# Linear attention and two gated MLP layers on one core: zeros, the order of step 0 and 1, alternating PSUM banks, and a first sum moved to GpSimd

## The reference

```python
kv = einsum('bhsd,bhse->bhde', k, v)              # 4 x 8 heads, 576 tokens, 64 wide
out = einsum('bhsd,bhde->bhse', q, kv)
rms = sqrt(mean(out * out, axis=-1) + 1e-06)
x = (out / rms * g_norm)  ->  [2304 tokens, 512]
h = x @ w_in1;  x = (h * sigmoid(1.702 * h)) @ w_out1     # w_in 512 x 2048, w_out 2048 x 512
h = x @ w_in2;  out = softplus(h) @ w_out2
```

## Time and profile before

| | |
|---|---|
| median of 3 runs | 817.93 us (817.62 to 819.13) |
| profiled execution | 818.39 us, span of instructions 816.6 us |
| TensorE matmul busy | 805.2 us, 99% of the span |
| TensorE weight load busy | 734.2 us |
| VectorE busy | 588.9 us |
| ScalarE busy | 425.0 us |
| GpSimd busy | 223.0 us |
| chain that ended last | TensorE 92%, VectorE 3%, ScalarE 2% |

### The profile page before, as it was taken

The page is one execution under the profiler, slowest core; times in us unless marked ns, Lnnn a source line. Parts: engine busy times, 40 slices in busy tenths (PEclk is TensorE's granted clock), DMA queues, the critical chain, the costliest instruction groups (busy, mean ns, idle before and its releaser), DMA issues.

```text
span 816.6 us, 12377 instructions
## 1 busy us (share of the span) xinstructions
PE 805.2 (99%) x4604; PEld 734.2 (90%) x4604; DVE 588.9 (72%) x1029; ACT 425.0 (52%) x809; POOL 223.0 (27%) x263
## 2 busy tenths in 40 slices
PE   8989999999999999999999999999999999999998
PEld 7978999999999999999998888898888988989886
DVE  3779767687665786665678777888767889766774
ACT  3773332334221233223246776788767678766765
POOL 4888987304421403254501401100000000000000
PEclk9999999999999999999999999999999999999999
DMA  9936547426455462756642525224433322452402
GB/s 358 405 158 236 213 143 280 159 116 217 159 219 203 154 238 91 246 200 250 231 171 101 206 102 205 107 90 150 164 126 119 152 91 101 159 180 90 149 33 77
DMA packets 24426, 139.78 MB, mean 171 GB/s; under 512 B 2224, under 2 KB 6960, under 8 KB 17200
## 3 DMA queue, kind: packets, MB, share of 16 engines
q1 hardware_dynamic: 24224, 138.95, 46.6%
q10 hardware_dynamic: 144, 0.07, 0.0%
HBM read 104.92 MB, written 34.08 MB: 170 GB/s over the span
## 4 chain that ended last, share of the span: by engine, by line
PE 92%; DVE 3%; ACT 2%; issue 1%; DMA 1%; SPq 0%; ACTq 0%; DVEq 0%
PE ps L640 42%; PE ps L705 23%; PE ps L713 16%; PE ps L710 8%; PE ps L583 1%; DMA kv_in_sb<-k_v 1%; PE ps L566 1%; DVE xs_f L984 1%; DVE gs_f L1013 1%; PE ps L602 0%; DVE ex L1066 0%; DVE rms L953 0%; PE ps L588 0%; DVE gs_f L1069 0%; ACT fix L819 0%
## 5 line engine op out<-in xcount | busy, mean ns | idle before, releaser
L640 PE MATMUL ps<-xs,w_in 128*128 128x384 f32 x2016 | 409.5, 338 | 2.3 <-DVE gs_f L1013 2.0
L640 PEld LDWEIGHTS ps<-xs,w_in 128*128 128x128 f32 x2016 | 356.4, 188 | 27.7 <-issue 4.0
L705 PE MATMUL ps<-w_out,gs 128*128 128x512 f32 x864 | 226.0, 393 | 0.0
L1013 DVE TENSOR_TENSOR gs_f<-ps,gs_f 128x384 f32<-128x384 f32 x240 | 133.2, 555 | 113.7 <-PE ps L640 112.2
L705 PEld LDWEIGHTS ps<-w_out,gs 128*128 128x128 f32 x864 | 160.0, 188 | 23.9 <-issue 0.5
L713 PE MATMUL ps<-gs,w_out 128*128 128x512 f32 x576 | 148.2, 392 | 0.0
L713 PEld LDWEIGHTS ps<-gs,w_out 128*128 128x128 f32 x576 | 105.6, 188 | 16.4
L809 ACT ACTIVATE lg<-gs_f 128x384 f32<-128x384 f32 x73 | 38.3, 526 | 123.2 <-DVE gs_f L1013 122.1
L487 POOL TENSOR_TENSOR w_in<-w_in_f,w_in 128x256 fp32r<-128x256 f32 x112 | 94.1, 876 | 29.1 <-ACT w_in L849 28.9
L844 ACT CAST gs<-gs_f 128x384 fp32r<-128x384 f32 x96 | 48.9, 509 | 67.7 <-DVE gs_f L1073 66.4
L710 PE MATMUL ps<-gs,w_out 128*128 128x256 f32 x576 | 83.9, 281 | 0.1
(11 more groups left out here) (64 smaller groups left out, 576.8 us busy)
## 6 DMA issues: line engine op xcount, KB each, us to landing
w_in<-w_kept SPq DMA_DIRECT2D x40, 1792.0 KB, 7.3
w_kept<-w_in SPq DMA_DIRECT2D x16, 1792.0 KB, 10.8
w_in_f<-w_in SPq DMA_DIRECT2D x16, 512.0 KB, 4.1
w_out_f<-w_out SPq DMA_DIRECT2D x16, 512.0 KB, 9.0
kv_in_sb<-k_v SPq DMA_DIRECT2D x8, 640.0 KB, 10.2
kv_in_sb<-k_v SPq DMA_DIRECT2D x8, 576.0 KB, 11.9
q_sb<-q_t SPq DMA_DIRECT2D x16, 288.0 KB, 10.2
out<-xy SPq DMA_DIRECT2D x18, 256.0 KB, 7.8
```

Of the source, the lines that this page charges most:

```text
L640: mm = nc.tensor.matmul(ps[:, bank, 0:HALF], w[:, wp, W_OF[k], cols], xs[:, k, xp, t], start=(new and t == 0 and (wp, xp) == (HI, HI)), st ...
L705: mm = nc.tensor.matmul(ps[:, acc_bank(1, j), 0:DM], g[:, j * P:(j + 1) * P], w, start=new, stop=done)
L1013: nc.vector.tensor_tensor(to, bank, other, ALU.add).then_inc(added, 1)
```

## The change

1. After raw_output(0) TensorE multiplies five more zeros.
2. Banks alternate: in odd steps BANK_A and BANK_B change places (bank_a, bank_b). P1 of step m then waits only for C21_ADD of step m - 1, and P6 for C12_ADD.
3. product(1, P1) is issued between turn(15) and product(0, P3). The counts of prod_done follow (products_done, step_done).
4. hidden(0, C21) moves on ScalarE ahead of the last gain, and on VectorE the whole gate of C21 stands ahead of C12_ADD in step 0.
5. x's first sums: T1 on VectorE behind unit 8 (it needs x_made 6), T3 on GpSimd (first_t3), T2 on VectorE behind unit 10, where it waits for T3, and T4 behind unit 11.
6. GpSimd's queue: x_early(B21) ahead of w_sums(1), then w_high(1), w_low(1), x_early(B22), first_t3, x_early of T1, T3, T2, T4. The wait for the split of step 0's C21 stands ahead of w_sums(2) instead of behind it.

```diff
         def products_done(m, k):
-            place = {P2: P6, P6: P2}.get(k, k) if m == 0 else k
+            place = {P2: P6, P6: P2, P3: PRODUCTS}.get(k, k) if m == 0 else -1 if (m, k) == (1, P1) else k
             return PRODUCTS * m + place + 1
-        X_EARLY = (B11, B21, B22, T3, T2, T4, T1)
+        X_EARLY = (B11, B21, B22, T1, T3, T2, T4)
+        X_EARLY_SUMS = (T1, T2, T4)
+            def first_t3():
+                a, b, op = x_sum_of(0, T3)
+                nc.gpsimd.tensor_tensor(x_sum(0, T3), a, b, op).then_inc(t3_early, 1)
             x_early(B11)
+            x_early(B21)
             w_sums(1)
-            x_early(B21)
             w_high(1)
             w_low(1)
-            for slot in X_EARLY[2:]:
+            x_early(B22)
+            first_t3()
+            for slot in X_EARLY[3:]:
                 x_early(slot)
             w_out_low(0, 0)
+            pool.wait_ge(g_split, C21 + 1)
             w_sums(2)
-            pool.wait_ge(g_split, C21 + 1)
             w_high(2)
-                bank = BANK_B if k in (P6, P7, P4) else BANK_A
+                bank = bank_b(m) if k in (P6, P7, P4) else bank_a(m)
                     if m > 0:
-                        pe.wait_ge(added, ADDS * (m - 1) + C12_ADD + 1)
+                        pe.wait_ge(added, ADDS * (m - 1) + C21_ADD + 1)
+                if k == P6 and m > 0:
+                    pe.wait_ge(added, ADDS * (m - 1) + C12_ADD + 1)
                 raw_output(u)
+                if u == 0:
+                    zeros(5)
             turn(UNITS - 1)
+            product(1, P1)
             product(0, P3)
@@ ScalarE
+                if u == UNITS + 1:
+                    hidden(0, C21)
                 if u >= TURN_LAG:
                     gain(u - TURN_LAG)
@@ VectorE
-                if slot == T2:
+                if slot == T2 and ci == 0:
+                    dve.wait_ge(t3_early, 1)
+                elif slot == T2:
                     dve.wait_ge(x_raw_made, x_raws(ci, T3))
-                if u == 2 * PAIRS + 1:
-                    dve.wait_ge(x_made, 2 * PAIRS)
-                    raw_x(0, T3)
+                if u == 2 * PAIRS:
+                    dve.wait_ge(x_made, PAIRS + 2)
+                    raw_x(0, T1)
+                if u == 2 * PAIRS + 2:
                     raw_x(0, T2)
-                if u == 2 * PAIRS + 2:
+                if u == 2 * PAIRS + 3:
                     raw_x(0, T4)
-                if u == 2 * PAIRS + 3:
-                    raw_x(0, T1)
                 if m == 0:
                     gate_split(m, C11)
-                    add(m, C12_ADD)
                 if phase:
                     softplus(m, C21)
                 else:
-                    gate_product(m, C21)
-                    if m > 0:
-                        gate_split(m, C21)
-                if m > 0:
-                    add(m, C12_ADD)
+                    gate(m, C21)
+                add(m, C12_ADD)
                 if ends:
                     low_x(ci + 1, T2)
-                if m == 0:
-                    gate_split(m, C21)
```

More of the change, by code:

```diff
@@ L153, in build @@
         x_raw_made = sem("x_raw_made")
+        t3_early = sem("t3_early")
         x_hi_made = sem("x_hi_made")
@@ L234, in build, with bank_a, bank_b, step_done @@
         P1_UNIT, P2_UNIT = 10, 12
+        def bank_a(m):
+            return BANK_B if m % 2 else BANK_A
+        def bank_b(m):
+            return BANK_A if m % 2 else BANK_B
         def products_done(m, k):
-            place = {P2: P6, P6: P2}.get(k, k) if m == 0 else k
+            place = {P2: P6, P6: P2, P3: PRODUCTS}.get(k, k) if m == 0 else -1 if (m, k) == (1, P1) else k
             return PRODUCTS * m + place + 1
+        def step_done(m):
+            return max(products_done(m, k) for k in range(PRODUCTS))
         def split_buffer(d):
@@ L302, in x_raws @@
         def x_raws(ci, slot):
-            return 4 * ci + X_RAW_ORDER.index(slot) + 1
+            if ci == 0:
+                return X_EARLY_SUMS.index(slot) + 1
+            return len(X_EARLY_SUMS) + 4 * (ci - 1) + X_RAW_ORDER.index(slot) + 1
         def x_his(ci, slot):
@@ L399, in load_raw @@
                     if last is not None:
-                        sp.wait_ge(prod_done, PRODUCTS * (last + 1))
+                        sp.wait_ge(prod_done, step_done(last))
                     sp.wait_ge(w_stored, 16 * ((last if last is not None else d - 1) + 1))
@@ L738, in _ @@
                 for k in range(PRODUCTS):
-                    product(m, k)
+                    if (m, k) != (1, P1):
+                        product(m, k)
                     down(m - 1, came, shares(m)[k])
@@ L787, in first_product @@
                     wait_down(act, m - 2)
-                nc.scalar.copy(hid(m, C21), ps[:, BANK_A, 0:HALF]).then_inc(t1_made, 1)
+                nc.scalar.copy(hid(m, C21), ps[:, bank_a(m), 0:HALF]).then_inc(t1_made, 1)
             def keep_c11():
@@ L801, in hidden @@
                     act.wait_ge(prod_done, products_done(m, P2))
-                    h = ps[:, BANK_A, 0:HALF]
+                    h = ps[:, bank_a(m), 0:HALF]
                 else:
@@ L916, in _ @@
                     round_x(ci + 1, T3)
-                hidden(m, C21)
+                if m > 0:
+                    hidden(m, C21)
                 if ends:
@@ L991, in add @@
             def add(m, which):
-                a, b = ps[:, BANK_A, 0:HALF], ps[:, BANK_B, 0:HALF]
+                a, b = ps[:, bank_a(m), 0:HALF], ps[:, bank_b(m), 0:HALF]
                 p1 = hid(m, C21)
@@ L1039, in hidden_of @@
             def hidden_of(m, tile):
-                return ps[:, BANK_A, 0:HALF] if tile == C11 and m > 0 else hid(m, tile)
+                return ps[:, bank_a(m), 0:HALF] if tile == C11 and m > 0 else hid(m, tile)
             def gate(m, tile):
```

## The result

| | before | after |
|---|---|---|
| median | 817.78 us (817.58 to 819.13, 8 runs) | 822.12 us (819.31 to 823.34, 8 runs) |
| ratio, with its 95% interval | | 1.0044 (1.0032 to 1.0057) |
| profiled execution | 818.39 us, span 816.6 | 822.84 us, span 821.0 |
| VectorE busy, GpSimd busy | 588.9, 223.0 us | 583.6, 225.6 us |

By the medians the change costs 4.3 us, not the 2.3 of the forecast; it lands near the 821.8 of the first rival. The ratio is not the quotient of the medians (1.0053) but an estimate from all executions; it puts the cost at 3.6 us, with 2.6 to 4.7 as its interval. The spans of the two profiled executions differ by 4.4 us, which is where the places can be read.

The account below looks back on a forecast made before the run. Only matmul time bounds TensorE from 64 us on, so edits count in the first 64 us or where another engine stops it. 0.4 us gained up to down(0), 2.7 lost at down(1): +2.3 on 817.93 makes 820.2, range 818.0 to 823.0.

Parts of the forecast that it names:

- rival 1: At down(1): the clock falls in the new TensorE wait of some 2 us; +3.9, 821.8 us, chance 0.22.
- Zeros: First stage: five more zeros hold the clock, 1.6 us saved, but transfers let unit 8 gain at most 0.55.
- Rival 4: First stage: the zeros don't hold the clock, x_made 4 not earlier, 0.6 more; +2.9, 820.8 us, chance 0.08.
- Wait (b): Attention: three raw_output waits for VectorE's scale, 1.8 us together; not saved but replaced, P6 1.1 us later.
- GpSimd in the first stage: Attention: GpSimd idles ahead of B21, then becomes the bound; P6 at 52.05 instead of 50.94, 1.1 us later.
- Products: Up to down(0): products' order gains 1.5 us, less GpSimd's 1.1; down(0) at 62.95 instead of 63.38, 0.4 gained.
- T0: End of step 0's gates: the moment C21 is split, forecast at 62.9 us against 63.3 before.
- GpSimd behind T0: From T0 to down(1): 2.97 us of sums precede a 15.17 us chain; down(1) +1.8 to +2.8, taken as +2.3.
- Rivals 2: At down(1): no wait if GpSimd's collisions stay under 0.4 us; -0.4, 817.5 us, chance 0.07.
- rival 3: Attention: GpSimd isn't the bound, T0 3.3 us earlier, sums behind T0 still cost 2.7; -0.6, 817.3 us, chance 0.07.
- the two together: Attention and down(1): GpSimd isn't the bound and no wait at down(1); -3.5, 814.4 us, chance 0.06.
- if half clock follows the wait: Behind down(1)'s forecast TensorE wait of 2 to 3 us: a sign that would show the forecast wrong.

Follow-up runs that it names:

- e6_zeros_only: The kernel before with the five zeros and nothing else; 818.06 us, ratio 1.0001.
- e2_b21_back: The changed kernel with w_sums(1) ahead of x_early(B21) again in GpSimd's queue; 818.89 us, ratio 1.0003.
- e1_sums_back: The changed kernel with w_sums(2) put back ahead of the wait for C21's split; 818.68 us, ratio 1.0005.
- e8_zeros_products: The changed kernel with GpSimd's queue and x's first sums as before, keeping zeros, alternating banks, P1 ahead of P3 and C21 ahead; 817.08 us, ratio 0.9985.
- e4_fill: The changed kernel with 13 matmuls of unread result in TensorE's wait ahead of down(1); 820.35 us, ratio 1.0025.
- e5_only_sums_late: The kernel before with only the wait for C21's split moved ahead of w_sums(2); 820.78 us, ratio 1.0041.
- e10_fill_both: The changed kernel with filler matmuls in both new waits, 11 ahead of raw_output(13) and 13 ahead of down(1); 819.89 us, ratio 1.0020.
- c_after: The changed kernel run again as it is, beside other experiments on one chip; 822.01 us, ratio 1.0040 against the kernel before.
- e3_both_back: The changed kernel with w_sums(1) ahead of B21 and w_sums(2) ahead of the wait for C21's split again; 816.01 us, ratio 0.9973.

## Why the forecast was right in its places and short in its size

**Zeros: right.** 0.41 us of waiting is left of 1.69, the rows behind it are at full speed (1.16 for the 1.96 of the earlier trace rows), and unit 8 starts at 26.26 where 26.25 was said. The granted clock of the 12th us is 1.00 where it was 0.50:

```profile
12.00:13.00 1.00, 1.00 (x16) 0.88 (x16) 0.84 (x2) 0.23 (x2) 1.00 (x1) 1.00 1.07 421
```

That the transfers leave 0.55 of the 1.6 in the trace is shown by e6_zeros_only; in the median it is 0.2. Rival 4 fell.

**Wait (b) replaced, not saved: right.** VectorE stands still for T3, and its own row for the next sum is

```profile
42.24 1.55 DVE L1020 TENSOR_TENSOR xs_f<-xs_f,xy 128x768 f32<-128x768 f32 x1 [2.21 <-POOL xs_f L529]
```

TensorE waits 1.96 us at raw_output(13) instead of three times for 1.8. e2_b21_back shows the cause: with the old order of GpSimd's queue the wait is gone.

**GpSimd in the first stage: right.** Forecast and trace: B21 at 25.0 (24.79), T3's sum done at 42.5 (40.38 + 1.82 = 42.20), its price 1.8 (1.82), T1's low part at 45.9 (43.06 + 2.40 = 45.46), T2's low part at 52.0 (49.58 + 1.81 = 51.39). P6 at 52.05 came true as 52.07, but not for the stated reason alone: in this execution GpSimd was done 0.7 us before, and TensorE was itself late, with raw_output(13) at the slower clock. In e1_sums_back, at full clock, P6 starts at 51.73 behind GpSimd's subtraction. So the reason holds at full clock, 0.3 us earlier than said, and the fall of the clock filled the difference. The chain was priced well because each item of it had a row of its own kind.

**Products: right.** P5 was said for 58.5 and starts about a product behind 57.24, by estimate at 58.3. T0 was said for 62.9; the split of C21 is

```profile
61.94 0.56 DVE L1093 TENSOR_TENSOR gs<-gs_f,gs 128x384 fp32r<-128x384 f32 x1
```

so T0 is 62.50, and down(0) starts at 62.60 after 0.38 us (62.95 after 0.4 was said). e8_zeros_products confirms a gain from this order, 1.3 us with the zeros, where the forecast counted 0.4 in all because GpSimd's 1.1 was taken off it.

**GpSimd behind T0: right in its chain, with some luck in its time.** The chain ended at 81.21 where 81.1 was said: it began 0.4 earlier and was 0.5 longer, since w_sums(2) took 3.63 (62.58 to 66.21) instead of 2.97, taking turns with VectorE. The wait is 2.53 (2.4), down(1) starts 2.07 later than before, inside the 1.8 to 2.8. (The forecast's own chain, 81.1, gives +1.9; it took 2.3, the middle of its bounds.) That it lies inside is in part luck: about 0.5 of the 2.07 is the fall of the clock in attention, for which the forecast had no term, and in e4_fill, where that fall is missing, down(1) starts 1.57 later. There T0 is at 62.0, 0.9 earlier than said. e1_sums_back and e5_only_sums_late show the cause from both sides, once by undoing the edit and once by doing it alone: 3.3 us less, and 2.35 us more at full clock. Rivals 2 and 3 fell. (The -3.5 of the two together doesn't follow from rival 3's terms, -0.6 and -2.7, which make -3.3.)

**The clock: the term that was mis-sized.** The sum had no term for it; it stood as rival 1, at 0.22, with "dense matmuls on both sides" against it. Among the signs of being wrong the forecast named "if half clock follows the wait", and half clock did follow it: by its own sign the forecast failed here. Of the 13 executions of the changed kernel 11 had a mean granted clock of 0.997 or less, and the time follows the clock: 819.31 and 819.89 at 0.999, 820.72 to 821.20 at 0.997, 822.01 to 823.34 at 0.995 and 0.996. Dense matmuls on both sides of the wait did not protect here; the matmuls that e4_fill and e10_fill_both put into it do. Rival 1's figure of 821.8 is near the 822.1 measured, but its place was too narrow: it counted a fall at down(1) only. e4_fill, which prevents that one, gives back 1.7 us, and e10_fill_both, which prevents the one behind raw_output(13) as well, 2.1. The forecast had said that this wait replaces the old ones and had left out that one wait of 2 us is not the same as three of 0.5 to 0.8: in the kernel before nothing is slow behind those. At full clock the change costs 1.6 us (e10_fill_both against the kernel before beside it), where 2.3 was forecast, and the falls of the clock add 2.1, where nothing was: one term was 0.7 too dear and another missing, and the two errors partly cancel. That the forecast's 820.2 is close to e10_fill_both's 819.9 is luck as well, since the kernel before had 818.29 there and not the 817.93 that the forecast started from.

**Behind down(1): nothing gives time back**, as said. What was read in the 403rd us (0.75) is a late transfer in one execution and not an effect that was shown to belong to the change.

What stays open: what decides, from one execution to the next, whether the clock falls behind a wait. No run here controls it, apart from filling the wait.

## What to carry to other kernels

An engine that never shows in the waits of the bounding engine can still have no slack: add up its queue from its last release to the next thing that is needed of it (here 15.2 of 15.8 us), and don't put a wait ahead of work that until then ran in someone else's shadow. A change of several parts should be tried part by part, since edits that gain 2.4 us together were here covered by two bad lines of one queue: 822.0 with them, 816.0 without. And a single wait of 2 us on TensorE is to be priced with a probable half clock behind it, or be filled with matmuls that nobody reads.

## What was unexpected of the hardware

- **Half clock behind 2 us of standing still, amid dense matmuls.** Behind waits of 1.96 to 2.53 us the granted clock fell to 0.50, once with 0.62 as the mean of the first us, and the fall cost 1.5 us at down(1); 11 of 13 executions had a mean clock of 0.997 or less. The profiled execution of the kernel before shows it behind its 1.69 us at the start. By their mean clocks about a third of its executions had such a fall, and their median is only 0.2 to 0.6 us above the others' (818.51 against 818.30 and 817.94), as transfers set the pace there.
- **Filling the wait holds the clock.** Thirteen matmuls of 384 columns took 2.42 us in e4_fill, and the rows behind them are at full speed. down(1) still waited 0.31 us for GpSimd behind them, so they delayed nothing.
- **A fall behind a long wait is not certain.** In the profiled execution of e1_sums_back TensorE waited 2.2 us at raw_output(13) and had a mean clock of 1.000; c_after, with 2.4 at the same place, went down to 0.50. Length alone doesn't decide it: in the profiled execution of after 1.96 us at the same place were enough.
- **VectorE and GpSimd take turns by instruction, in both directions.** VectorE's sum of two SBUF tiles took 1.55 us at 42.24, while GpSimd's cast and subtraction stood around it, against the 0.96 of the earlier trace rows; GpSimd's subtraction took 2.40 instead of 1.82. Even so, rearranging x's first sums with T3's on GpSimd, at 1.82 us for 0.96, gained 1.1 us (e3_both_back against e8_zeros_products); the three waits for VectorE's scales, 1.8 us in e8_zeros_products, are gone in e3_both_back. The Trainium skill (Perfetto Trace Analysis, Optimizing Scalar/DVE Operations) says that such offloading might not help because of the shared port; the trace agrees as far as the taking of turns goes (1.55 for 0.96, 2.40 for 1.82), but here the offloading came with a gain, in a queue of GpSimd that still had room. What it is worth in the changed kernel's fuller queue was not run.
